# Expert weights rounded in another order, two transposes moved forward, and half as many scatters in flight

## What is computed

```python
def _moe2_ref(x, w_gate, w_local, w1, w2):       # x: 4 x 576 tokens of 512
    logits = np.einsum('bsd,de->bse', x, w_gate)
    local_gate = 1.0 / (1.0 + np.exp(-np.einsum('bsd,de->bse', x, w_local).squeeze(-1)))
    for b in range(B):
        prev_e = -1
        for s in range(S):
            fresh_e = int(np.argmax(logits[b, s]))
            if s == 0 or local_gate[b, s] < 0.5:
                e = fresh_e
            else:
                e = prev_e if prev_e >= 0 else fresh_e
            prev_e = e
            ls = logits[b, s] - logits[b, s].max()
            p = np.exp(ls)
            p /= p.sum() + 1e-09
            h = np.maximum(x[b, s] @ w1[e], 0.0)  # w1[e]: 512 x 1024, w2[e]: 1024 x 512
            out[b, s] = p[e] * (h @ w2[e])
```

## Time and profile before

| | us |
|---|---|
| median of 3 runs | 532.31 (531.90 to 532.61) |
| the profiled run | 531.9 |
| its span | 530.2 |
| expert stage, within the span | about 270 to 530 |

### The profile page before, as it was taken

How to read it: one execution, slowest core, us unless ns; L and a number is a source line. 1 busy time by engine, 2 the same in 40 slices (tenths; PEclk the granted TensorE clock), 3 DMA queues, 4 the chain that set the end, 5 groups by cost and what they waited for, 6 DMA issues and landing times. The chain is left out here.

```text
span 530.2 us, 13320 instructions
## 1 busy us (share of the span) xinstructions
PE 510.3 (96%) x5374; PEld 431.7 (81%) x5374; DVE 301.5 (57%) x492; ACT 261.8 (49%) x450; POOL 220.5 (42%) x224
## 2 busy tenths in 40 slices
PE   6999999999999999999999999999999999999993
PEld 5898999988989999678887787888887777888872
DVE  4686878878986554287505657422375578522231
ACT  2555676666786331564625556322555557422330
POOL 3069999999999950436620001100111011100001
PEclk9999999999999999999999999999999999999998
DMA  8466464654510000006669399111382977111101
GB/s 298 133 201 208 139 227 157 203 189 139 165 70 1 0 1 1 1 1 205 253 239 337 106 351 339 61 40 40 102 295 50 348 278 265 41 40 42 53 25 43
DMA packets 31351, 75.34 MB, mean 142 GB/s; under 512 B 4159, under 2 KB 4415, under 8 KB 31296
## 3 DMA queue, kind: packets, MB, share of 16 engines
q1 hardware_dynamic: 25600, 60.37, 33.8%
q0 software_dynamic: 3104, 9.46, 4.6%
q10 hardware_dynamic: 2592, 4.74, 3.1%
HBM read 57.46 MB, written 17.55 MB: 141 GB/s over the span
## 5 line engine op out<-in xcount | busy, mean ns | idle before, releaser
L568 POOL TENSOR_TENSOR gate<-gate,tap 128x576 f32<-128x576 f32 x64 | 93.1, 1455 | 5.3
L612 POOL DMA_INDIRECT out_rows<-o_sb,meta_cur x18 | 18.6, 1033 | 151.5 <-DVE o_sb L1448 151.5
L1435 DVE TENSOR_TENSOR h_t<-pair_ps,h_t 128x512 fp32r<-128x512 f32 x36 | 24.9, 691 | 88.5 <-ACT h_t L1175 88.5
L662 PE MATMUL turn<-wts,h_t 128*128 128x512 f32 x144 | 60.0, 417 | 1.4 <-issue 1.4
L662 PE MATMUL num_ps<-wts,y_t 128*128 128x512 f32 x144 | 59.5, 413 | 0.1
L663 PE MATMUL turn<-wts,h_t 128*128 128x512 f32 x144 | 56.9, 395 | 0.0
L663 PE MATMUL num_ps<-wts,y_t 128*128 128x512 f32 x144 | 56.9, 395 | 0.0
L664 PE MATMUL turn<-wts,h_t 128*128 128x512 f32 x144 | 56.9, 395 | 0.0
L664 PE MATMUL num_ps<-wts,y_t 128*128 128x512 f32 x144 | 56.9, 395 | 0.0
L1209 DVE TENSOR_REDUCE absmax<-pair_ps 128x8 f32<-128x1024 f32 x31 | 38.0, 1225 | 29.8 <-PE pair_ps L671 29.8
L1167 ACT ACTIVATE h_sb<-num_ps 128x512 f32<-128x512 f32 x36 | 21.5, 598 | 65.6 <-PE num_ps L664 65.6
(11 more groups left out here) (210 smaller groups left out, 1117.6 us busy)
## 6 DMA issues: line engine op xcount, KB each, us to landing
ring<-in_w SPq DMA_DIRECT2D x36, 512.0 KB, 6.9
stage<-in_w SPq DMA_DIRECT2D x28, 512.0 KB
kq_t<-in_kq SPq DMA_DIRECT2D x15, 576.0 KB, 6.4
sorted_rows<-padrow SPq DMA_DIRECT2D x9, 771.0 KB, 5.7
v_sb<-in_v_aug SPq DMA_DIRECT2D x16, 325.0 KB, 3.2
ysl<-sorted_rows ACTq DMA_DIRECT2D x18, 257.0 KB
wout_t<-in_w_out_t SPq DMA_DIRECT2D x1, 1024.0 KB, 7.9
wval_sb<-in_w_val SPq DMA_DIRECT2D x1, 1024.0 KB, 9.5
```

What stands on the lines that cost most here:

```text
L568: nc.gpsimd.tensor_tensor(g, g, tap[:, t % 2, :], ALU.add).then_inc(conv_step, 1)
L662: nc.tensor.matmul(dst, x[0], w[0], start=first, stop=False)
```

## The change

It has four parts. `SENT` goes from 6 to 3. In expert 0's first tile `turn_y` and `turn_few` go ahead of the wait for the second half of `h_t`, that is behind `down(3)`. ScalarE takes chunks 0 and 1 ahead of the first half, chunk 2 behind the first ReLU, 3 to 5 behind the next rows, 6 and 7 at the end of the expert; in expert 0's first tile six chunks instead of five. VectorE takes chunks 0, 1 and 2 ahead of the first half, none between the halves, 3 to 5 behind the next rows, 6 and 7 at the end; in expert 0's first tile chunk 0 ahead of `o_sb` and 1 to 5 behind it.

```diff
-        SENT = 6
+        SENT = 3
@@ each_expert
-                for i in chunks[5:]:
+                for i in chunks[6:]:
                     split(i)
@@ TensorE, tile_of
                 down(3)
+                if not early:
+                    turn_y(t + 1)
+                    turn_few()
                 pe.wait_ge(ht_ok, t * 2 + 2)
                 for kk in range(4, KT):
                     ins = down(kk)
-                    if not early and kk == KT - 3:
-                        turn_y(t + 1)
                 ins.then_inc(o_ok, 1)
-                if not early:
-                    turn_few()
@@ ScalarE, tile_of
-                for i in [] if begins else chunks[0:1]:
+                for i in [] if begins else chunks[0:2]:
                     round_weights(i)
...
-                        for i in chunks[1:2]:
+                        for i in chunks[2:3]:
                             round_weights(i)
...
-                    for i in chunks[0:2]:
+                    for i in chunks[0:3]:
                         round_weights(i)
-                for i in chunks[2:5]:
+                for i in chunks[3:6]:
                     round_weights(i)
@@ VectorE, tile_of
-                for i in [] if begins else chunks[0:1]:
+                for i in [] if begins else chunks[0:3]:
                     rest_of_weights(i)
                 for half in range(2):
-                    if half == 1 and not begins:
-                        for i in chunks[1:2]:
-                            rest_of_weights(i)
...
-                for i in [] if begins else chunks[2:5]:
+                for i in chunks[0:1] if begins else chunks[3:6]:
                     rest_of_weights(i)
                 dve.wait_ge(meta_ok, t + 1)
                 dve.wait_ge(o_ok, t + 1)
                 V.tensor_scalar(o_sb[:], turn_ps[1][:], meta_cur[:, 1:2], None, ALU.mult).then_inc(o_read, 1)
-                for i in chunks[0:5] if begins else []:
+                for i in chunks[1:6] if begins else []:
                     rest_of_weights(i)
```

## The result

The changed kernel takes 537.04 us (median of 7 runs, 534.52 to 538.55), the kernel before beside it 532.31 (7 runs, 531.22 to 533.87). The ratio is **1.0088, with a 95% interval of [1.0064, 1.0111]**: slower, as forecast, but by 4.7 us instead of 2.4. That is the very edge of the range: 0.04 above its 537.0 by the median, 536.99 by the ratio. The profiled run took 537.73 us, its span is 535.9 against 530.2. So 5.7 us of span have to be found.

The account below looks back on a forecast made before the run. TensorE, busy 510.3 of 530.2 us, was taken as the bound. Terms of -0.8, 0, +3.2 and 0 gave +2.4 us: 534.3 from the profiled run, 534.7 us after allowing for the median; range 532.4 to 537.0.

Parts of the forecast that it names:

- a rival in which the scatters alone cost up to 3 us: Scatters held up by `SENT` 3, so TensorE waits at `turn_few`: 537.7 us at half the bound, 541 in full; chance 0.12.
- What bounds the kernel: TensorE, busy 510.3 of 530.2 us; other engines' changes count only through a wait of TensorE.
- Unit costs: Per weight chunk: 0.95 us for ScalarE's rounding, 1.13 us for VectorE's rest.
- Part 1: Expert 0's first tile: earlier turning removes most of a 1.8 us ReLU wait, VectorE takes half back; gain 0.8 us.
- Part 2: ScalarE's new chunk order between experts: the ReLU starts when it did; zero.
- Part 3: VectorE's longer list ahead of `h_t` at first tiles of experts 2, 3, 6 (t3, t8, t12): 3.2 us; few-row tiles zero.
- the sign to look for at t8: At expert 3's first tile, TensorE would wait 1.0 us before the first `down`.
- Part 4: `SENT` 6 to 3: scatters spread out under load, then catch up; last one at worst 0.3 us later; zero cost.
- The margin at `turn_few`: Expert 0's first tile: few rows there at 282.3, needed at about 282.65, a margin of 0.35 us.
- The rule "each microsecond beyond that is a microsecond of TensorE": Expert 0's first tile: lateness of the last scatter beyond the 0.35 us margin delays TensorE equally.
- the sum: -0.8 for earlier turning, +3.2 for VectorE's order, zero for ScalarE's order and `SENT`: +2.4 us.

Follow-up runs that it names:

- e4: The changed kernel with only `SENT` put back from 3 to 6; 535.29 us, ratio 1.0062 to the kernel before.
- e7: The changed kernel with `SENT` 6 and VectorE making one rest ahead of `h_t`, two between its halves; 529.41 us, ratio 0.9946 to the kernel before.
- e2: The kernel before with only `turn_y` and `turn_few` moved forward in expert 0's first tile; 531.33 us, ratio 0.9986.
- e8: e7 with chunks later still: none ahead of the first half on ScalarE, no rest ahead of `h_t` on VectorE; 531.62 us, ratio 0.9976 to the kernel before.
- e10: The kernel before with one more rest ahead of `h_t`, only in the first tile of expert 6 (t12); 534.08 us, ratio 1.0029.

## Why the prediction was right, and where it fell short

- **The number.** The direction and most of the mechanism were right; that the median lies at the range's very edge is luck. The upper end stood at 537.0 for the milder half of a rival in which the scatters alone cost up to 3 us. They cost 1.90, and the clock, which stood in no term, paid the rest; without its 1.55 us the kernel would have been at about 535.5.
- **What bounds the kernel.** Right. Each piece of the loss is a stretch of TensorE that waits or runs at the lower clock.
- **Unit costs** of 0.95 and 1.13 us. Right: 286.20 to 290.00 is four roundings, 321.24 to 326.91 five rests.
- **Part 1, -0.8.** Right in mechanism and size where the rows are there: 24.48 us to the first `down` in e4, against 24.42 by its steps. In the changed kernel the gain turned into +1.16, because the ground on which it stood ("at 282.2 the rows of t1 must be there") gave way.
- **Part 2, zero.** Right: TensorE has no new wait on ScalarE in the changed kernel, and e7 keeps that order and gains.
- **Part 3, +3.2.** Right: 1.10 at t3, 1.00 at t8, 1.13 at t12, and nothing at the tiles with few rows. Only the sign to look for at t8 was wrong: not 1.0 in brackets but 0.62, since brackets count from a modelled end.
- **Part 4, zero.** This is the step that failed, "so it has caught up by the fifteenth, at about 265", and with it "goes out at 271.2, at worst 0.3 us later". GpSimd was 3.8 us behind at the seventh scatter, about as the prediction had it, but the backlog didn't heal: the fifteenth went out at 268.53, 5.7 us later than before, and not at about 265. So the last scatters met the weight chunks issued from 265.88, the fourteenth landed only at about 275.0, and the last went out at 276.56. I had called the late stretch quiet, though the earlier trace rows show the second four chunks at 266.15, ahead of the last scatters. The margin at `turn_few` held: with `SENT` = 6 there is no wait (e2, e4), and by the landings there it is rather 0.6 to 0.9 us than 0.35. The rule "each microsecond beyond that is a microsecond of TensorE" held as well: SyncE was 2.4 us later and TensorE waited 1.7. The rival that had this (0.12) put 3 us on it. By the Trainium skill's rule used in the prediction, page "DMA: Bandwidth & Descriptors", section "Anatomy of one DMA — SWDGE (gpsimd) path", a scatter takes an estimated 2.6 us, and three in flight would be enough; the rows above disagree, with 8.7 us for one scatter beside the weights.
- **What the sum lacked.** The price of a wait was taken as the wait. Behind a wait of 1.8 us the granted clock can fall to 0.50, and the profiled run paid 1.55 us for that at t12. The earlier trace rows could not have warned: behind the wait of 1.81 before the change the clock stood at 1.00.

By its own terms, corrected: -0.26 for the earlier start of the stage, -0.74 for part 1 (24.48 - 25.22), +1.90 for part 4 on t0 and t1 (26.38 in the changed kernel less 24.48 in e4), +3.23 for part 3, +1.55 for the clock make 5.68 us. Of the rivals, one happened on top of the forecast and not in its place. Treating them as alternatives kept the range's centre too low: the changed kernel's median lies at the range's very edge.

## What to carry to other kernels

When a change moves a consumer forward and, elsewhere, makes its producer later, price the two together: here each costs nothing (0.9999 and 0.9986), and the pair costs 1.9 us, the clock's part included. Weight preparation that stands ahead of a short step on the critical chain costs its full length once that chain has no slack, so put it behind the step: one, two or three rests ahead of `h_t` made 0.9946, 0.9981 and 1.0062 here. Moving it still later (e8) did not pay. And where TensorE has to wait for about 2 us in otherwise dense work, count the lower clock behind the wait too (about 1.6 us where the traces show it, in about half of e10's runs), or give it small products to do meanwhile.

## What the hardware did that I had not expected

- **The clock after a short wait.** After waits of 1.83 and 1.84 us, one of 2.75 us, and a pair of 0.85 and 1.20 us, TensorE's granted clock fell to 0.50 for some 3 to 4 us. After others of the same length (1.81 in the kernel before, 1.84 at t3 in the changed one, 1.83 at t12 in e4) it stayed at 1.00. In e10 it fell in about half of the runs. What decides it in a given run stays open; it cost 1.55 us in the changed kernel's trace and 1.57 in e10's. The Trainium skill, page "TensorE: Matmul & The Clock Gate", section "HAM oscillation — how this bites in real kernels", counts such a stretch at half of its duration as lost; the windows agree, with 1.7 us of lost clock and 1.55 us of lost time.
- **One scatter, three durations.** The same 128 rows took 3.5 us at most from issue to release in the changed kernel's last scatter (276.56 to 280.04), 6.4 in the kernel before, and 8.7 beside four fresh weight chunks.
- **Hold-ups without a releaser** in the third product of the first half of `up`, 0.2 to 1.7 us, in some kernels and not in others. Nothing in these runs explains them.
